# Earlier row loads, five y buffers, zeros in mid unit and an earlier first product copy in a fused attention, mixture-of-experts and feed-forward kernel

## The reference, cut to what matters

```python
# 1 retention attention, float32: q, k, v are (4, 8, 576, 64)
scores = scale * (q @ k.T);  ret = scores * Dmat;  x = ret @ v        # -> x (2304, 512)
# 2 mixture of experts: 8 experts, 512 -> 1024 -> 512, the best two per token
for e in range(E):
    for k in range(2):
        mask = top2[:, k] == e
        h = np.maximum(x[mask] @ w1[e], 0.0)
        out[mask] += top2_w[mask, k, None] * (h @ w2[e])
# 3 feed-forward 512 -> 2048 -> 512
h = x @ w_in
return (h * np.cos(h)) @ w_out
```

## Time and profile before

| what | value |
|---|---|
| median of 3 runs | 984.85 us (983.6 to 988.26) |
| profiled execution, its own time | 986.97 us |
| its span | 985.2 us |
| PE busy | 959.6 us, 97% |
| DVE, ACT, POOL busy | 57%, 48%, 10% |
| mean busy share of the DMA engines | highest in attention, under 90% in most slices behind it |

### The profile page before, as it was taken

One profiled execution on the slowest core, in us unless ns is written; L12 is line 12 of the kernel. 1 busy time (PEld: TensorE's weight loads), 2 busy tenths in 40 slices (PEclk: granted clock), 3 DMA queues, 4 the chain that ended last, 5 costly groups with the idle time before them and its releaser, 6 DMA issues.

```text
span 985.2 us, 17024 instructions
## 1 busy us (share of the span) xinstructions
PE 959.6 (97%) x6144; PEld 860.7 (87%) x6144; DVE 562.3 (57%) x1118; ACT 477.7 (48%) x889; POOL 94.7 (10%) x93
## 2 busy tenths in 40 slices
PE   8999999999999999999999999999999999999998
PEld 8888889898988989899998988988988888788887
DVE  4788644544545554433332145567777767776665
ACT  1445334343433443332333146556767766666555
POOL 2276500000000000000000032101100000000000
PEclk9999999999999999999999999999999999999999
DMA  9998455468688786764526248867764766556561
GB/s 364 345 321 303 173 203 202 160 236 310 262 270 329 265 322 229 256 248 150 192 67 231 86 137 304 289 252 289 265 240 167 291 256 235 184 216 249 228 235 54
DMA packets 79521, 231.92 MB, mean 235 GB/s; under 512 B 6880, under 2 KB 32736, under 8 KB 71264
## 3 DMA queue, kind: packets, MB, share of 16 engines
q1 hardware_dynamic: 73696, 212.20, 60.2%
q0 software_dynamic: 5760, 18.88, 5.2%
HBM read 168.14 MB, written 62.91 MB: 235 GB/s over the span
## 4 chain that ended last, share of the span: by engine, by line
PE 75%; SPq 6%; DMA 5%; ACT 5%; DVE 4%; issue 3%; POOL 1%; DVEq 0%; ACTq 0%; POOLq 0%
PE ps L1855 16%; PE ps L1666 13%; PE ps L1684 13%; PE ps L1841 12%; SPq L539 4%; PE ps L1771 3%; PE ps L1783 2%; PE ps L1819 2%; PE ps L1572 2%; PE ps L1610 2%; DMA gath<-x_slots 2%; PE ps L1587 2%; DMA y_slots<-y_sb 2%; PE ps L1638 2%; PE ps L1702 2%
## 5 line engine op out<-in xcount | busy, mean ns | idle before, releaser
L1666 PE MATMUL ps<-xs,w_hi 128*128 (+1 forms) x784 | 185.3, 316 | 0.0
L1855 PE MATMUL ps<-w_sb,g_hi 128*128 128x512 f32 x576 | 180.8, 395 | 0.1
L1272 DVE TENSOR_TENSOR w_lo<-raw,w_hi 128x1024 fp32r<-128x1024 f32 x48 | 58.8, 1226 | 159.2 <-ACT w_hi L794 159.2
L1666 PEld LDWEIGHTS ps<-xs,w_hi 128*128 128x128 f32 x784 | 135.3, 191 | 0.7
L1666 PE MATMUL ps<-xs,w_lo 128*128 (+1 forms) x392 | 122.5, 312 | 0.0
L1841 PE MATMUL ps<-x_odd,w_sb 128*128 128x320 f32 x672 | 118.7, 312 | 3.9 <-DVE angle L1442 1.8
L1841 PEld LDWEIGHTS ps<-x_odd,w_sb 128*128 128x128 f32 x672 | 107.4, 189 | 15.8 <-ACT p_sb L935 3.4
L794 ACT ACTIVATE w_hi<-raw 128x1024 fp32r<-128x1024 f32 x48 | 50.9, 1060 | 136.6 <-PE ps L1684 107.5
L1855 PE MATMUL ps<-w_sb,g_lo 128*128 128x512 f32 x288 | 112.7, 391 | 0.0
L1855 PEld LDWEIGHTS ps<-w_sb,g_hi 128*128 128x128 f32 x576 | 101.3, 188 | 9.8 <-issue 0.3
L716 POOL DMA_INDIRECT y<-y_slots,pos_i x36 | 34.9, 970 | 636.3 <-SPq L636 446.1
(11 more groups left out here) (193 smaller groups left out, 1615.8 us busy)
## 6 DMA issues: line engine op xcount, KB each, us to landing
w_sb<-w_pairs SPq DMA_DIRECT2D x24, 1792.0 KB
w_sb<-w_pairs SPq DMA_DIRECT2D x40, 1024.0 KB, 9.7
raw<-weights SPq DMA_DIRECT2D x64, 512.0 KB
w_pairs<-stage SPq DMA_DIRECT2D x24, 1024.0 KB, 7.1
y_slots<-zeros_sb SPq DMA_DIRECT2D x42, 256.0 KB, 4.1
gath<-x_slots SPq DMA_DIRECT2D x40, 256.0 KB, 7.1
y_slots<-y_sb SPq DMA_DIRECT2D x40, 256.0 KB, 2.1
qk<-qk SPq DMA_DIRECT2D x18, 512.0 KB
```

The lines of the kernel that those rows point to most:

```text
L1272: tt(w_lo[:, at], raw[:, f % 2, :], w_hi[:, at].bitcast(F32), ALU.subtract).then_inc(split_done, 1)
L1666: last_one = nc.tensor.matmul(ps[5 + half][:, 0:HALF], w[:, at:at + P], xs[:, bass.ds(g % 2, 1), a, k, half * HALF:(half + 1) * HALF].rear ...
L1855: last_one = nc.tensor.matmul(ps[j][:, :], a[:, slot % 2, part, j * C:(j + 1) * C], w2_sb[slot % 3][:, hl, part * DM:(part + 1) * DM], sta ...
```

## The change

The number of matmuls, activations and vector instructions stays. What moves:

1. **Units.** `NY` goes from 3 to 5, so each y tile has a buffer. In `unit_loads(g)` the first two row loads of the next unit come first, then the stores of unit g - 1, then the rest. The eight zero blocks are issued at step f = 4.
2. **First Strassen slot (8).** Its first product goes to ps7 and the turns of ps5 and ps6 shift by one, so the first three products wait for other things than before. `x2_high(1, 6)` and `x2_low(1, 6)` move from slot 7 into slot 8.
3. **Strassen slots.** `copy_p1(s)` stands before `cosine(s-1, 3)` on ACT.
4. **Block 0.** The transposes of tiles 3 to 5 and 6 to 7 move half a slot later on PE, and `prepare` and `combine` of tiles 3 to 5 stand between other steps of slots 1 and 2.
5. **Table.** Two groups of columns (`before`, `ones`) move from `table_sb` to the piece of `attn_table` that is loaded with `q_mixed`, a little later; waits on `q_mixed_in` are added.

```diff
-NY = 3
+NY = TPU
...
-                  ("q_mixed", PAIRS * C),
-                  ("ident", P), ("number", E), ("first", E), ("before", C), ("ones", C),
-                  ("half_pi", 1)):
+                  ("q_mixed", PAIRS * C), ("before", C), ("ones", C),
+                  ("ident", P), ("number", E), ("first", E), ("half_pi", 1)):
...
-            return ps[7] if i == 2 else ps[5 + i % 2]
+            if i in (2, 2 * FP):
+                return ps[7]
+            return ps[5 + (i + (i > 2 * FP)) % 2]
...
             def unit_loads(g):
...
+                for j in range(2):
+                    sp.wait_ge(tx_done, TPU * g + j + 1)
+                    sp.sem_inc(passed_sp, 1)
+                    load_rows(j, v_next)
+                for j in range(TPU):
+                    store_rows(g - 1, j)
                 for f in range(FE):
-                    if f < TPU:
+                    if 2 <= f < TPU:
...
+                    if isinstance(g, int) and g < E - 2 and f == 4:
+                        for j in range(E):
+                            zero_block(E * TPU + j + (g - 1) * E)
...
                 unit_loads(g)
-                for j in range(E):
-                    zero_block(E * TPU + j + (g - 1) * E)
-                for j in range(TPU):
-                    store_rows(g, j)
...
             def ahead(b, p):
                 first = FIRST_TILE[b + 1]
                 if b == 0:
-                    if p == 1:
-                        for j in range(3):
-                            prepare(first + j)
...
-                    if p == 7:
-                        x2_high(1, 6)
...
                 turn(slot, 1)
+                if slot == 1:
+                    prepare(FIRST_TILE[1])
                 cosine(slot, 1)
+                if slot == 1:
+                    prepare(FIRST_TILE[1] + 1)
+                    prepare(FIRST_TILE[1] + 2)
             for slot in range(FP, SLOTS + 1):
                 b, p = slot // FP, slot % FP
                 if slot == FP:
                     g_high(slot - 1, 1)
+                    if slot < SLOTS:
+                        copy_p1(slot)
+                    x2_high(1, 6)
                 else:
                     g_high(slot - 1, 2)
+                    if slot < SLOTS:
+                        copy_p1(slot)
                     cosine(slot - 1, 3)
-                if slot < SLOTS:
-                    copy_p1(slot)
-                if slot > FP:
                     g_high(slot - 1, 3)
...
+                    if slot == 2:
+                        combine(FIRST_TILE[1] + 1)
                     g_low(slot - 1, 1)
+                    if slot == 2:
+                        combine(FIRST_TILE[1] + 2)
...
                     drain(slot, 1, h_sb[0], p1_sb)
+                if slot == FP:
+                    x2_low(1, 6)
...
-                if slot == FP and o < 2:
-                    pe.wait_ge(g_done, i - 1)
+                if slot == FP and o == 0:
+                    pe.wait_ge(xT_copied, SIZES[1])
+                elif slot == FP and o < 3:
+                    pe.wait_ge(g_done, i - 2)
...
+                        if slot == 2 and part == 0:
+                            for j in range(3):
+                                transpose_x2(FIRST_TILE[1] + j)
+                        if slot == 4 and part == 0:
+                            for j in range(3, 5):
+                                transpose_x2(FIRST_TILE[1] + j)
```

More of the change, by code:

```diff
@@ L574, in store_pair @@
                     sp.dma_start(w2_pairs[i], stage2[i % 2][:, :, :].bitcast(F32)).then_inc(pair_out[i % 2], 16)
-            for j in range(TPU):
-                store_rows(0, j)
             def unit_loads(g):
@@ L608, in _ @@
                 unit_loads(g)
-                for j in range(TPU):
-                    store_rows(g, j)
+            for j in range(TPU):
+                store_rows(last - 1, j)
             def load_w1(slot):
@@ L632, in _ @@
                 store_rows(last, j)
-            for i in range(NY):
+            for i in range(FRONT[1]):
                 sp.wait_ge(y_out[i], last * (16 * y_buffer(i)[2]) + 16)
@@ L739, in softplus @@
                 act.wait_ge(logit_done, hi)
+                if k == 0:
+                    act.wait_ge(q_mixed_in, 16)
                 above(act, picked_done, k)
@@ L1460, in ahead @@
                 if b == 0:
-                    if p == 1:
-                        for j in range(3):
-                            combine(first + j)
                     if p == 3:
@@ L1478, in ahead @@
                             x2_low(1, at)
-                    if p == 7:
-                        x2_low(1, 6)
                 else:
@@ L1505, in _ @@
                 reduce(slot, 1)
+                if slot == 1:
+                    combine(FIRST_TILE[1])
             for slot in range(FP, SLOTS + 1):
@@ L1557, in count @@
                 pe.wait_ge(picked_done, k + 1)
+                if k == 0:
+                    pe.wait_ge(q_mixed_in, 16)
                 nc.tensor.matmul(bank[0:C, RANKS:RANKS + n * E], tab("before", C), picked[:, lo * E:hi * E],
@@ L1754, in transpose_x2 @@
                     pe.wait_ge(g_done, 3)
+                if n == FIRST_TILE[2]:
+                    pe.wait_ge(p1_copied, 1)
                 if n >= 6:
@@ L1877, in _ @@
                     first = FIRST_TILE[b + 1]
-                    if b == 0:
-                        if p == 1:
-                            for j in range(3):
-                                transpose_x2(first + j)
-                        if p == 3:
-                            transpose_x2(first + 3)
-                            transpose_x2(first + 4)
-                    elif p < 5:
+                    if 0 < b and p < 5:
                         transpose_x2(first + p)
```

## The result

The changed kernel takes 970.75 us (median of 4 runs, 970.46 to 971.42). The kernel before took 985.29 in the same comparison (983.60 to 988.26): ratio 0.985, 95% interval 0.9826 to 0.9875, 14.5 us less. The forecast was 970.8. In the profiled executions the span fell from 985.2 to 968.8, 16.4 us. Of the difference of 1.9 between these two drops, 1.7 is that the profiled execution of the kernel before took 986.97 us, more than its median.

A forecast was written before the change was run, and what follows sets the result against it. PE, busy 97%, was taken as the bound, so only its waits and slow-clock stretches could give time. 12.2 + 2.4 + 0.5 = 15.1 us off gave 971.9 or 969.8 by base; forecast 970.8, range 963 to 975 (8 in 10).

The forecast's parts named there:

- Unit starts: Starts of units: earlier row loads remove PE's waits for `gath` and the slow clock, 12.2 us saved.
- Zeros in mid unit: Zero blocks between weight loads 4 and 5: load 5 about 2 us late, covered by slack, 0 us.
- Rival 3: Mid-unit zeros starve the weight loads in five units and the kernel gets slower, 995 us at 5 each; chance 0.03.
- Transposes in block 0: Before slot 2: PE's wait for `combine` goes, 2.4 us saved (1.8 to 2.5); tiles 6 and 7 add nothing.
- Strassen stage: Slots 8 to 24: slot 8 gains 2.1 us, the early copy's toll takes most back, about 0.5 us saved.
- the 0.42 for each boundary: Early `copy_p1` delays the ACT and DVE chain 0.42 us at 15 slot boundaries, 6.3 in all, 3.8 absorbed.
- Table: Table columns loaded later with `q_mixed`: 0 us, as POOL already waited for that piece earlier.
- the two bases: Profiled execution 986.97 us and median 984.85; the sum gives 971.9 or 969.8, truth expected between because clock halving may vary.
- 1: Rival: the Strassen waits do go, 9.5 us more saved, 961 to 962 us; chance 0.17.
- 2: Rival: unit starts keep a wait, `w_high` waiting for the raw chunk; 6 us remain, 977 us; chance 0.12.
- 4: Rival: row load late for another reason, the 12.2 us stay, something else costs 2; 982 to 985 us; chance 0.04.

The follow-up runs named there:

- a_zeros16: Changed kernel with sixteen zero blocks in mid unit in units 1 and 3, none in 2 and 4, eight in 5: 972.39 us.
- a_copyback: Changed kernel with `copy_p1` back between the last cosine and `g_high` from slot 9 on: 974.13 us.
- a_zerosend: Changed kernel with the eight zero blocks back at the end of units 1 to 5: 976.63 us.
- a_again: Changed kernel measured once more, nothing edited: 971.74 us.
- a_tiles67: Changed kernel with the transposes of tiles 6 and 7 back at the end of slot 3: 973.62 us.
- a_copy9: Changed kernel with `copy_p1` early in slots 8 and 9 alone, in its old place from slot 10 on: 971.30 us.
- b_rows: Kernel before with only the next unit's first two row loads moved ahead of the stores; three y buffers, zeros at unit end: 992.67 us.
- a_slot8back: Changed kernel with slot 8's banks and the last `x2_high` and `x2_low` as before, `copy_p1` still early: 974.81 us.

## Why the prediction was right, and where it was not

**Unit starts, -12.2: right**, 12.7 measured. As forecast, PE had no wait between 180 and 500 us and the full clock, and the row loads left 14.5 us ahead of where PE takes them (289.78 less 275.28). What the text made too little of is that the order is only one of three keys, and the weakest: alone it costs 3.5 us. "That alone gives PE nothing", said of the five buffers, is wrong: alone they give 8.8, of which 5.7 are waits.

**Zeros in mid unit, 0: right, but not by its working.** The DMA share of 0.08 was the emptiest stretch near there: in the kernel before it was 1.01 from 242 to 249 us and 1.01 again from 264 to 268. What helped is that the eight blocks took SP 6.69 us in mid unit where they took 8.97 at the end, so that weight load 5 left 7.40 us behind load 4 (257.00 - 249.60), hardly late, and not 9.0. Only a_zeros16 used the slack, and twice the zeros cost 0.4 us. Rival 3 is out.

**Transposes in block 0, -2.4: mis-sized.** The local reading was right, 2.7 us at slot 2. The step that failed is what followed it: the sum took the gain at slot 2 to the end of the stage, and said of tiles 6 and 7 that their move "removes no wait and adds none". It did not ask whether the chain of ACT and DVE could follow, nor what the transposes of tiles 3 to 5 release on POOL. The stage gained 0.7; how the loss divides between the two stays open.

**Strassen stage, -0.5: mis-sized, 2.7 measured.** Its parts: slot 8 gave 2.2 (2.1 forecast), 1.3 of it the lower clock. The early copy was to cost the chain 6.3 less 3.8 by slot 24; measured, it gains 0.4 in all. The forecast left 0.5 us at the second product of slot 24; it came 2.6 earlier after S (219.77, before 222.36). The term that failed is the 0.42 for each boundary. Here is ACT in the changed kernel at the boundary of slots 13 and 14, to be read beside the earlier trace rows:

```profile
718.16 0.47 ACT L952 ACTIVATE turns<-h_sb 128x320 f32<-128x320 f32 x1
...
719.13 0.42 ACT L940 ACTIVATE p_sb<-ps 128x320 f32<-128x320 f32 x1
719.45 0.46 ACT L958 ACTIVATE angle<-angle 128x320 f32<-128x320 f32 x1
...
721.46 0.47 ACT L952 ACTIVATE turns<-h_sb 128x320 f32<-128x320 f32 x1
```

The two `turn` rows of the kernel before at the same boundary:

```profile
734.34 0.47 ACT L947 ACTIVATE turns<-h_sb 128x320 f32<-128x320 f32 x1
...
737.39 0.47 ACT L947 ACTIVATE turns<-h_sb 128x320 f32<-128x320 f32 x1
```

The copy is recorded with 0.42, but the next instruction starts 0.32 behind its start, and the round from one `turn` to the next is 3.30 (721.46 - 718.16) where before it was 737.39 - 734.34 = 3.05, a toll of 0.25. The same round at all fifteen boundaries grew by 2.4 us in sum, not 6.3: 0.25 at eight of them, less at the others, and at two it shrank by 0.2. Against that, DVE's waits for PE on the Strassen products fell from 3.8 us to 0.4. From slot 12 to slot 24 the changed kernel loses 0.3 us to a_copyback (165.26 between their second products, against 164.92), and it had won 0.7 from S to slot 12 (54.51 against 55.19); the 0.4 is what remains. The rest of the picture held: the waits for p_sb are gone, waits for h_sb stand in their place, and block 2 is not shorter (the second products of slots 21 and 24 are 41.94 us apart, before 41.90).

**Table: 0**, but it is not idle: it frees the room for the two more buffers.

**The sum.** By the profile 15.1 was forecast and 16.4 came: units +0.5 and the start +0.3, block 0 -1.7, Strassen +2.2. Two errors of about 2 us cancelled. That the forecast of 970.8 fell within 0.1 us of the median is luck. By the medians the drop was 14.5, 0.6 less than the sum, and the base that the forecast implies, 985.9, was 0.6 above the 985.29 measured; these cancelled too. The reason given for standing between the two bases bears out: the clock of slot 8 does vary between executions with the same code.

**Rivals.** 1 (all Strassen waits go) did not come, nor 2 and 4. Yet 2 had a mechanism that exists: with the zeros at the end of the unit `w_high` does wait for the raw chunk and PE behind it (a_zerosend, 5.7 us).

## What to carry to other kernels

Where several edits all lie on one wait, run each alone before you name the cause: here the zeros' move alone gave 10.9 of 12.7 us, the buffers alone 8.8, and the one with the best story did harm alone, since with three buffers what delays the stores holds up the copies behind which `relu` stands. Look at the granted clock of both sides before you put a whole difference down to a wait. When a step is moved later, list what its semaphore releases on every engine, the one that issues gathers too, and see when that is needed next. The ACT copy put on the chain here lengthened a boundary by some 0.25 us at most, and not by its recorded 0.42.

## What the hardware showed that I had not expected

The start varies by more than any term of the sum but that of the unit starts. PE waits there for the first row loads, and the clock granted after that wait differs. The window from 126 to 129 us in the changed kernel, in a_again and in a_tiles67 (same code ahead of it), by columns as above:

```profile
126.00:129.00 3.00, 2.93 (x15) 1.00 1.00 382
```

```profile
126.00:129.00 3.00, 2.79 (x9) 0.57 0.98 362
```

```profile
126.00:129.00 3.00, 2.53 (x10) 0.50 0.91 302
```

The waits ahead of them were 0.69 and 1.26, 1.82 and 1.00, 2.71 and 0.47 us. The length of a wait alone does not decide whether the clock falls: a_copy9 waited 1.82 and 1.22 at the same place and kept 1.00, and four waits of 2.2 us in b_rows, in units 2 to 5, left the clock at 1.00 from 200 to 500 us, while 1.81 us in slot 8 of a_slot8back were followed by 0.57. What decides it stays open.
